# Another order of the loads, the weight splits and the mask copies at the start of a fused linear-attention and feed-forward kernel

## Chip, cores and metric

The kernel runs on one core of a Trainium2 chip. The metric is the device time in microseconds of one execution; lower is better. Times given are medians of several runs.

## The reference

Inputs are q, k, v and f_logit of shape (4, 8, 768, 48), and two pairs of weights, w_in (384, 2048) and w_out (2048, 384), all float32.

```python
# gated linear attention, a recurrence over time t
f = 1 / (1 + exp(-f_logit))
for t in range(S):
    state = f[:, :, t, :, None] * state + einsum('bhd,bhe->bhde', k[:, :, t], v[:, :, t])
    y[:, :, t] = einsum('bhd,bhde->bhe', q[:, :, t], state)
x = y.transpose(0, 2, 1, 3).reshape(B * S, H * D)          # 3072 tokens x 384
# feed-forward layer 1: ELU
h = x @ w_in1;  g = where(h > 0, h, exp(min(h, 0)) - 1);  x = g @ w_out1
# feed-forward layer 2: squared ReLU
h = maximum(x @ w_in2, 0);  out = (h * h) @ w_out2
```

## The kernel before

The sequence is cut into NC = 6 chunks of C = 128 steps. A unit (c, h) is chunk c of two of the four batches (h is 0 or 1), so there are twelve units, each with eight heads per batch. Within a unit the decayed score matrix is built in seven levels l = 0 to 6: product(c, h, l) on TensorE (PE) multiplies keys by queries of neighbouring blocks of width 2**l. After each level the queries and keys are multiplied by running products of the gates (q_update and own_k_update on VectorE, DVE; k_update on GpSimd, POOL; double makes the next products of the gates), and take (DVE, a masked copy, levels 0 to 4) and take5 and take6 (ScalarE, ACT) move the scores from PSUM to the tile PT; in the units of chunk 0 take4 on ACT does level 4. Then come transpose_keys, krow_copy (ACT), new_state (keys times values), q_state (queries times the old state), values (scores times values, padded into vz by pad_v), state_update (DVE) and last_column. Units (0, 0) and (0, 1) come first by themselves, with no feed-forward work beside them, as there is no attention output yet.

The first feed-forward layer works on tiles of 512 tokens in steps f = 0 to 15. hidden(c, f) is nine 512-column matmuls (each float32 operand is held as a high and a low float32r half: three products for three blocks of channels), output(c, f) nine more. Between them: hidden_copies (ACT: Exp into e, Relu into g), activate (DVE), high (ACT, makes ghi) and low (DVE or POOL, makes glo). The attention of chunk c is interleaved with the feed-forward of chunk c - 1 in half-step slots by feed(c, h, slots): first_period and second_period are the two halves for c = 1, period(c, h) the pattern for c = 2 to 5. After that feed_forward runs what is left of layer 1 and layer 2.

Weights of layer 1 come as 32 chunks of 128 x 384, alternately from w_in and w_out. load_weights on SyncE (SP) loads them, split_weights on ACT makes the high half, split_weights on DVE the low half. Chunks 0 to 11 (STAGED) go to the tile stage, which lies where xhi, xlo, e, g and others are later; so first_x_split, which writes xhi, waits for the low halves of all twelve. Later chunks pass through the four buffers of raw, and load_weights waits there for the low half of chunk i - 4. split_at(1, f) says which chunks ACT splits after step f of chunk 1.

Each engine runs its own queue in the order in which its block of the program is written; there is no planner. Semaphores tie them: s_mm counts finished level products, and `level(s_mm, c, h, l)` is the wait for product(c, h, l); s_kT the transposed keys, s_u new_state, s_inter q_state, s_last the last columns. `taken(c, h, n)` is the wait for the first n takes of a unit. For the units from (1, 1) on product(c, h, l) with l = 1 or 2 waits for l takes:

```python
elif l in (1, 2):
    pe.wait_ge(*taken(c, h, l))
```

group(c, h, i) (L1318) on PE is product(c, h, 4 + i) followed by product(c, h + 1, i), where group(1, 1, i) takes the first product of unit (1, 2) as h + 1 = 2.

SP issues all loads of q, k, gates and values. load_v(c, h) loads values for new_state, load_staged_v(c, h) the same values for pad_v. The loads wait for their buffers: load_gates(c, h) for level 0 of unit h - 2 to be done with them, load_k for s_kT, load_q for s_inter, load_v and load_staged_v for s_u.

Of the kernel before, what the change touches and what calls it, by code (L numbers as in the profile page):

```python
# [40 lines left out]
STAGED = 12  # L41
# [60 lines left out]
def attention(nc, blk, sb, sem, ffn, stage, PT, ps, qk, fl, vn, w1, x2, ident_d, mask_d):  # L102
# [47 lines left out]
    s_kT, s_krow = sem("k_transposed"), sem("krow_ready")  # L150
# [9 lines left out]
    def level(sems, c, h, l):  # L160
        if second(c, h):
            return (sems[2], l + 1) if l < EARLY else (sems[3], l - EARLY + 1)
        before = max(2 * c + h - 1, 0)
        if l < EARLY:
            return sems[0], before * EARLY + l + 1
        short = 1 if before and (sems is s_q or sems is s_d) else 0
        return sems[1], before * LATE - short + l - EARLY + 1
# [114 lines left out]
    def more(c, h, n=1):  # L282

        return 2 * c + h + n < UNITS

    @blk.sync
    def _(sp):
        def load_gates(c, h):

            if past(c, h, 2):  # L290
                sp.wait_ge(*level(s_q, c, h - 2, 0))
                sp.wait_ge(*level(s_k, c, h - 2, 0))
                sp.wait_ge(*level(s_d, c, h - 2, 0))
            sp.dma_start(gate[:, h % 2, :].rearrange("p (u n) -> p u n", u=UB),
                         fl[bass.ds(c * B + 2 * h, UB), :, :].rearrange("u p n -> p u n")).then_inc(s_f[h % 2], 16)

        def load_q(c, h):

            if past(c, h, 4):
                sp.wait_ge(s_inter, count(c, h, 1, -3))  # L300
            elif past(c, h, 3):
                sp.wait_ge(*level(s_mm, c, h - 2, LEVELS - 1))
            if past(c, h, 3):
                sp.wait_ge(s_ql, count(c, h, 1, -1))
            for u in range(UB):
                sp.dma_start(queries(c, h)[:, u * PAIRS:(u + 1) * PAIRS, 1:C + 1],
                             qk[bass.ds(c * B + (2 * h + u), 1), :, 0:W]
                             .rearrange("g p (a t) -> p (g a) t", a=PAIRS)).then_inc(s_q_in[h % 2], 16)

        def load_k(c, h):  # L310

            if past(c, h, 3):
                sp.wait_ge(s_kT, count(c, h, 1, -1))
            sp.dma_start(keys_of(c, h).rearrange("p (u n) -> p u n", u=UB),
                         qk[bass.ds(c * B + 2 * h, UB), :, W:2 * W].rearrange("u p n -> p u n")).then_inc(s_k_in[h % 2], 16)

        def load_v(c, h):

            if past(c, h, 2):
                sp.wait_ge(s_u, count(c, h, 1, 0))  # L320
            sp.dma_start(v(c, h), vn[bass.ds(c * B + 2 * h, UB), :, :]
                         .rearrange("u s n -> s u n")).then_inc(s_v[h % 2], 16)

        def load_staged_v(c, h):

            if past(c, h, 2):
                sp.wait_ge(s_u, count(c, h, 1, 0) if past(c, h, 3) else 1)
            for u in range(UB):
                sp.dma_start(staged_v(c, h)[HP * (1 - u):HP * (2 - u), :, :],
                             vn[c * B + (2 * h + u), :, :].rearrange("(z s) n -> s z n", z=2)).then_inc(s_vs[h % 2], 16)  # L330

        def load_weights(chunks):
            for i in chunks:
                if i >= STAGED + 4:
                    sp.wait_ge(s_wlo[i % 2], (i - 4) // 2 + 1)
                sp.dma_start(w1_raw(i), w1[chunk_at(i), :, :]).then_inc(w1_loaded(i)[0], 16)

        def period(c, h):
            if more(c, h, 2):
                load_gates(c, h + 2)  # L340
                load_k(c, h + 2)
                load_q(c, h + 2)
            if more(c, h):
                sp.wait_ge(*level(s_mm, c, h + 1, 4))
                load_v(c, h + 1)
                load_staged_v(c, h + 1)

        def first_period():
            sp.wait_ge(*level(s_mm, 1, 0, 1))
            load_weights(range(18, 20))  # L350
            load_gates(1, 2)
            sp.wait_ge(*level(s_mm, 1, 0, 2))
            load_staged_v(1, 0)
            load_weights(range(20, 22))
            sp.wait_ge(*level(s_mm, 1, 0, 4))
            load_weights(range(22, 24))
            load_v(1, 0)
            sp.wait_ge(*level(s_mm, 1, 1, 1))
            load_gates(1, 3)
            load_weights(range(24, 26))  # L360

        def second_period():
            load_k(1, 2)
            load_q(1, 2)
            load_v(1, 1)
            load_staged_v(1, 1)
            load_weights(range(26, 30))
            sp.wait_ge(*level(s_mm, 1, 2, 0))
            load_weights(range(30, 32))
            load_k(1, 3)  # L370
            load_q(1, 3)
            sp.wait_ge(*level(s_mm, 1, 2, 4))
            load_v(1, 2)
            load_staged_v(1, 2)

        load_q(0, 0)
        sp.dma_start(gate[:, 0, W:2 * W], fl[1, :, :]).then_inc(s_f[0], 16)
        load_q(0, 1)
        sp.dma_start(ident[:], ident_d).then_inc(s_ident, 16)
        sp.wait_ge(*level(s_mm, 0, 0, 0))  # L380
        load_gates(1, 0)
        sp.wait_ge(*level(s_mm, 0, 0, 1))
        load_gates(1, 1)
        load_weights(range(1))
        sp.wait_ge(*level(s_mm, 0, 0, 2))
        load_q(1, 0)
        sp.wait_ge(*level(s_mm, 0, 1, 1))
        load_weights(range(1, 2))
        load_staged_v(0, 0)
        sp.wait_ge(*level(s_mm, 0, 0, 4))  # L390
        load_staged_v(0, 1)
        load_v(0, 0)
        sp.wait_ge(*level(s_mm, 0, 0, 5))
        load_weights(range(2, 4))
        sp.wait_ge(*level(s_mm, 0, 0, 6))
        load_v(0, 1)
        load_k(1, 0)
        load_weights(range(4, 6))
        sp.wait_ge(s_y, 1)
        load_weights(range(6, STAGED))  # L400
        sp.wait_ge(s_last, 1)
        load_weights(range(STAGED, FIRST_SPLIT))
        sp.wait_ge(s_last, 2)
        load_q(1, 1)
        load_k(1, 1)
        load_weights(range(16, 18))
        first_period()
        second_period()
        for c in range(2, NC):
            for h in range(2):  # L410
                period(c, h)

    @blk.scalar
    def _(act):
# [210 lines left out]
                    .to_broadcast([HP, n, X, 32]), ACT.Copy).then_inc(s_mask, 1)  # L625
        gates(0, 1, True)
        gates(1, 0, True)
        gates(1, 1, True)
        split_weights(range(0, 1))
        nc.scalar.activation(warm[:, 1:2], warm[:, 0:1], ACT.Exp)  # L630
        split_weights(range(1, 2))
        pad_v(0, 0)
        take4(0, 0)
        take5(0, 0)
        pad_v(0, 1)
        take4(0, 1)
        take6(0, 0)
        take5(0, 1)
        split_weights(range(2, 4))
        take6(0, 1)  # L640
        krow_copy(0, 0)
        split_weights(range(4, 7))
# [114 lines left out]
    def _(dve):  # L757
# [179 lines left out]
        def first_period():  # L937
# [26 lines left out]
            rest(1, 1, 0)  # L964
            activate(1, 5)
            low(1, 5)
            q_update(1, 0, 5)
            own_updates(1, 1, 1)
            take(1, 1, 1)
            activate(1, 6)  # L970
            double(1, 0, 5)
            double(1, 1, 1)
            low(1, 6)
            q_update(1, 0, 6)
            own_updates(1, 1, 2)
            split_weights(split_at(1, 5))
            activate(1, 7)
            rest(1, 0, 6)
            rest(1, 1, 2)
# [4 lines left out]
        def second_period():  # L984
            activate(1, 8)
            low(1, 8)
            state_update(1, 0)
            activate(1, 9)
            low(1, 9)
            split_weights(split_at(1, 9))  # L990
            activate(1, 10)
            q_update(1, 1, 4)
            own_updates(1, 2, 0)
            low(1, 10)
            rest(1, 1, 4)
            take(1, 2, 0)
            activate(1, 11)
            double(1, 2, 0)
            q_update(1, 1, 5)
            own_updates(1, 2, 1)  # L1000
            low(1, 11)
            take(1, 2, 1)
            activate(1, 12)
            double(1, 1, 5)
            double(1, 2, 1)
            low(1, 12)
            own_updates(1, 2, 2)
            own_k_update(1, 1, 6)
            take(1, 2, 2)
            split_weights(range(28, 29))  # L1010
            activate(1, 13)
            low(1, 13)
            double(1, 2, 2)
            q_update(1, 1, 6)
            double(1, 1, 6)
            step(1, 2, 3)
            activate(1, 14)
            low(1, 14)
            split_weights(range(30, 31))
            state_update(1, 1)  # L1020
            split_weights(range(29, 32, 2))

        nc.vector.memset(e[:, 0, :], 0.0).then_inc(s_warm, 1)
        for which in "YA":
# [740 lines left out]
```

## Time and profile before

| | |
|---|---|
| Time, median of 3 runs | 972.11 us (971.56 to 974.31) |
| Profiled execution, its own time | 971.56 us |
| Its span, first to last instruction | 969.8 us |
| Mean granted clock of TensorE | 0.982 |
| PE busy | 951.4 us (98%), 11636 matmuls |
| DVE busy | 504.0 us (52%) |
| ACT busy | 402.8 us (42%) |
| POOL busy | 236.8 us (24%) |
| Chain that ended last | PE 97%, DMA 1%, DVE 1%, issue 1% |

The table is read as follows. Busy time is the time in which an engine executed; register, branch and DMA-issuing instructions don't count. The chain that ended last is followed back from the last instruction, at each step to what released it. "Issue" is time in which an engine waited for nothing that the profile shows. The granted clock is TensorE's clock as a share of full speed.

### The profile page before, as it was taken

To read this page: it belongs to the slowest core of one execution; us is meant where nothing else is said; L and a number is where in the kernel's file an instruction comes from. 1 tells how busy PE (TensorE), PEld (TensorE's weight loads), DVE (VectorE), ACT (ScalarE), POOL (GpSimd) and SP (SyncE) were. 2 spreads that over 40 slices of the span, in tenths; PEclk is the share of its full clock that TensorE was granted. 3 is DMA by queue.
4 is the path that set the end of the run, shared out by engine and by line. 5 is a ranking of instruction groups with operands and counts; after the bars stand their busy time and mean duration, and the time that the engine had idled before them with its cause. 6 is when DMAs were issued, how large, how long until landed. Compare 5 with 4: busy or idle time off the path is not lost.

```text
span 969.8 us, 27529 instructions
## 1 busy us (share of the span) xinstructions
PE 951.4 (98%) x11636; PEld 785.4 (81%) x11636; DVE 504.0 (52%) x746; ACT 402.8 (42%) x706; POOL 236.8 (24%) x193
## 2 busy tenths in 40 slices
PE   6899999999999999999999999999999999999998
PEld 5778787887887888888878888888888888888897
DVE  7788577576666656572326653343343433433432
ACT  4656545353534543453444452242332422423322
POOL 3102216354545445454424550000000000000000
PEclk6789999999999999999999999999999999999999
DMA  7552312212121211110203331002020030020100
GB/s 238 164 158 91 110 50 86 79 45 79 56 79 45 71 63 57 46 67 3 66 2 122 98 102 37 1 14 53 0 54 11 0 64 1 9 56 0 21 14 33
DMA packets 72428, 56.88 MB, mean 59 GB/s; under 512 B 37249, under 2 KB 64641, under 8 KB 72321
## 3 DMA queue, kind: packets, MB, share of 16 engines
q1 hardware_dynamic: 69472, 43.87, 16.6%
q10 hardware_dynamic: 2848, 11.44, 3.3%
q8 instruction: 85, 1.39, 0.6%
q14 instruction: 23, 0.18, 0.1%
HBM read 45.84 MB, written 9.44 MB: 57 GB/s over the span
## 4 chain that ended last, share of the span: by engine, by line
PE 97%; DMA 1%; DVE 1%; issue 1%; ACT 0%; SPq 0%; DVEq 0%
PE ps L1667 8%; PE ps L1663 8%; PE ps L1662 8%; PE ps L1137 8%; PE ps L1686 7%; PE ps L1682 7%; PE ps L1683 7%; PE ps L1276 6%; PE ps L1299 6%; PE ps L1278 6%; PE ps L1285 6%; PE ps L1301 6%; PE ps L1305 5%; PE ps L1206 2%; PE ps L1172 1%; PE ps L1154 1%
## 5 line engine op out<-in xcount | busy, mean ns | idle before, releaser
L1607 DVE TENSOR_TENSOR g<-g 128x512 f32<-128x512 f32 x96 | 66.8, 696 | 240.9 <-ACT g L1522 240.3
L1522 ACT ACTIVATE g<-ps 128x512 f32<-128x512 f32 x112 | 67.0, 598 | 276.9 <-PE ps L1667 272.6
L688 POOL TENSOR_TENSOR glo<-g,ghi 128x512 fp32r<-128x512 f32 x65 | 89.6, 1379 | 194.3 <-ACT ghi L513 194.3
L1662 PE MATMUL ps<-xhi,wts 128*128 128x512 f32 x336 | 130.9, 390 | 0.0
L1663 PE MATMUL ps<-xhi,wts 128*128 128x512 f32 x336 | 130.9, 390 | 0.0
L872 DVE SCALAR_TENSOR_TENSOR g<-e,g 128x512 f32<-128x512 f32 x80 | 57.8, 723 | 136.7 <-ACT g L507 136.7
L1682 PE MATMUL ps<-ghi,wts 128*128 128x512 f32 x294 | 114.4, 389 | 0.0
L1683 PE MATMUL ps<-ghi,wts 128*128 128x512 f32 x294 | 114.4, 389 | 0.0
L506 ACT ACTIVATE e<-ps 128x512 f32<-128x512 f32 x80 | 47.8, 598 | 158.7 <-PE ps L1285 158.7
L1276 PE MATMUL ps<-xhi,wts 128*128 128x512 f32 x240 | 98.9, 412 | 0.2 <-ACT g L507 0.2
L1278 PE MATMUL ps<-xhi,wts 128*128 128x512 f32 x240 | 94.7, 395 | 0.3 <-issue 0.3
L1667 PE MATMUL ps<-xlo,wts 128*128 128x512 f32 x336 | 94.6, 390 | 0.0
L1299 PE MATMUL ps<-ghi,wts 128*128 128x512 f32 x234 | 93.8, 401 | 0.0
L1618 DVE TENSOR_TENSOR glo<-g,ghi 128x512 fp32r<-128x512 f32 x112 | 89.3, 798 | 5.6 <-ACT ghi L1529 5.1
L1301 PE MATMUL ps<-ghi,wts 128*128 128x512 f32 x234 | 91.3, 390 | 0.0
L1686 PE MATMUL ps<-glo,wts 128*128 128x512 f32 x294 | 82.8, 390 | 0.0
L1137 PEld LDWEIGHTS ps<-q,k 48*63 48x63 f32 (+6 forms) x4576 | 68.6, 134 | 17.4 <-issue 16.3
L1137 PE MATMUL ps<-q,k 48*63 48x32 f32 (+6 forms) x4576 | 74.7, 219 | 1.3 <-DVE PT L828 1.1
L1667 PEld LDWEIGHTS ps<-xlo,wts 128*128 128x128 f32 x336 | 63.1, 188 | 13.5 <-DVE xlo L865 0.3
L1662 PEld LDWEIGHTS ps<-xhi,wts 128*128 128x128 f32 x336 | 63.0, 188 | 13.1 <-ACT xhi L498 0.2
L513 ACT ACTIVATE ghi<-g 128x512 fp32r<-128x512 f32 x80 | 50.5, 631 | 55.6 <-DVE g L872 55.5
L1663 PEld LDWEIGHTS ps<-xhi,wts 128*128 128x128 f32 x336 | 63.1, 188 | 12.6
(132 smaller groups left out, 1555.8 us busy)
## 6 DMA issues: line engine op xcount, KB each, us to landing
raw<-w SPq DMA_DIRECT2D x52, 192.0 KB, 2.4
q<-qk SPq DMA_DIRECT2D x22, 256.0 KB, 3.7
gate<-fl SPq DMA_DIRECT2D x10, 512.0 KB, 4.4
k<-qk SPq DMA_DIRECT2D x10, 512.0 KB, 3.7
x<-xo ACTq DMA_DIRECT2D x6, 768.0 KB, 3.3
xs<-x ACTq DMA_DIRECT2D x6, 768.0 KB, 4.4
v<-vn SPq DMA_DIRECT2D x11, 384.0 KB, 3.6
krow<-vn SPq DMA_DIRECT2D x20, 192.0 KB, 4.5
```

The costliest lines, as they stand in the source:

```text
L688: nc.gpsimd.tensor_tensor(out=glo[:, f % 2, :], in0=g[:, f % 2, :], in1=ghi[:, f % 2, :].bitcast(F32), op=ALU.subtract).then_inc(s_glo, 1)
L1137: last = nc.tensor.matmul(to, k_all[rows, at * C + HP * z:at * C + HP * z + m], there, start=True, stop=True)
L1276: nc.tensor.matmul(ps[:, HID, :], wts[:, f, 0, m * P:(m + 1) * P], xhi[:, m, :], start=(m == 0), stop=False)
L1278: nc.tensor.matmul(ps[:, HID, :], wts[:, f, 1, m * P:(m + 1) * P], xhi[:, m, :], start=False, stop=False)
L1299: nc.tensor.matmul(ps[:, ACC + m, :], wts[:, n, 0, m * P:(m + 1) * P], ghi[:, f % 2, :], start=start, stop=False)
L1301: nc.tensor.matmul(ps[:, ACC + m, :], wts[:, n, 1, m * P:(m + 1) * P], ghi[:, f % 2, :], start=False, stop=False)
L1662: nc.tensor.matmul(h, w(0, k), xhi[:, k, :], start=(k == 0), stop=False)
L1663: nc.tensor.matmul(h, w(1, k), xhi[:, k, :], start=False, stop=False)
L1667: last = nc.tensor.matmul(h, w(0, k), xlo[:, k, :], start=False, stop=(k == KD - 1))
L1682: nc.tensor.matmul(acc[m], w(0, m), ghi[:, f % 2, :], start=start, stop=False)
L1683: nc.tensor.matmul(acc[m], w(1, m), ghi[:, f % 2, :], start=False, stop=False)
L1686: last = nc.tensor.matmul(acc[m], w(0, m), glo[:, f % 2, :], start=False, stop=stop)
```

## The change

Four functions get another order. No instruction is added or removed, apart from waits.

- SP, the opening: the twelve staged chunks are loaded in pairs from product(0, 0, 1) on; before, chunks 0 and 1 were loaded early, 2 to 5 about the ends of unit (0, 0)'s levels, and 6 to 11 after unit (0, 0)'s values. q and k of unit (1, 0) come after the last levels.
- SP, first_period: staged values and values of unit (1, 0) first, gates of unit (1, 2) after product(1, 0, 3) instead of product(1, 0, 1).
- SP, second_period and period: the wait for level 4 of the next unit ahead of load_v is gone, and load_q comes behind the values.
- ACT, the opening: chunks 0 to 3 are split earlier.
- DVE, first_period: chunks 22 and 23 are split after low(1, 5), not after own_updates(1, 1, 2); take(1, 1, 1) comes after activate(1, 6), not before.
- DVE, second_period: chunks 28 and 29 are split before activate(1, 11); take(1, 2, 1) comes after activate(1, 12), not before; 30 and 31 are split before low(1, 13), not at the end. (rest is take, where the level has one on DVE, and then double.) For unit (1, 2) level 0, take and double now both come before activate(1, 11).

```diff
--- before.py
+++ after.py
@@ -336,25 +336,27 @@
                 sp.dma_start(w1_raw(i), w1[chunk_at(i), :, :]).then_inc(w1_loaded(i)[0], 16)
 
         def period(c, h):
+            f = 8 * h
             if more(c, h, 2):
                 load_gates(c, h + 2)
+            if more(c, h, 2):
                 load_k(c, h + 2)
-                load_q(c, h + 2)
             if more(c, h):
-                sp.wait_ge(*level(s_mm, c, h + 1, 4))
                 load_v(c, h + 1)
                 load_staged_v(c, h + 1)
+            if more(c, h, 2):
+                load_q(c, h + 2)
 
         def first_period():
             sp.wait_ge(*level(s_mm, 1, 0, 1))
+            load_staged_v(1, 0)
             load_weights(range(18, 20))
+            sp.wait_ge(*level(s_mm, 1, 0, 2))
+            load_v(1, 0)
+            load_weights(range(20, 22))
+            sp.wait_ge(*level(s_mm, 1, 0, 3))
             load_gates(1, 2)
-            sp.wait_ge(*level(s_mm, 1, 0, 2))
-            load_staged_v(1, 0)
-            load_weights(range(20, 22))
-            sp.wait_ge(*level(s_mm, 1, 0, 4))
             load_weights(range(22, 24))
-            load_v(1, 0)
             sp.wait_ge(*level(s_mm, 1, 1, 1))
             load_gates(1, 3)
             load_weights(range(24, 26))
@@ -368,10 +370,9 @@
             sp.wait_ge(*level(s_mm, 1, 2, 0))
             load_weights(range(30, 32))
             load_k(1, 3)
-            load_q(1, 3)
-            sp.wait_ge(*level(s_mm, 1, 2, 4))
             load_v(1, 2)
             load_staged_v(1, 2)
+            load_q(1, 3)
 
         load_q(0, 0)
         sp.dma_start(gate[:, 0, W:2 * W], fl[1, :, :]).then_inc(s_f[0], 16)
@@ -380,24 +381,29 @@
         sp.wait_ge(*level(s_mm, 0, 0, 0))
         load_gates(1, 0)
         sp.wait_ge(*level(s_mm, 0, 0, 1))
+        load_weights(range(0, 2))
+        sp.wait_ge(*level(s_mm, 0, 0, 2))
+        load_staged_v(0, 0)
         load_gates(1, 1)
-        load_weights(range(1))
-        sp.wait_ge(*level(s_mm, 0, 0, 2))
-        load_q(1, 0)
-        sp.wait_ge(*level(s_mm, 0, 1, 1))
-        load_weights(range(1, 2))
-        load_staged_v(0, 0)
+        sp.wait_ge(*level(s_mm, 0, 0, 3))
+        load_weights(range(2, 4))
+        sp.wait_ge(*level(s_mm, 0, 1, 2))
+        load_weights(range(4, 6))
         sp.wait_ge(*level(s_mm, 0, 0, 4))
         load_staged_v(0, 1)
+        load_weights(range(6, 7))
+        sp.wait_ge(*level(s_mm, 0, 1, 3))
+        load_weights(range(7, 9))
+        sp.wait_ge(*level(s_mm, 0, 0, 5))
+        load_weights(range(9, 10))
         load_v(0, 0)
-        sp.wait_ge(*level(s_mm, 0, 0, 5))
-        load_weights(range(2, 4))
-        sp.wait_ge(*level(s_mm, 0, 0, 6))
+        sp.wait_ge(*level(s_mm, 0, 1, 4))
+        load_weights(range(10, STAGED))
+        sp.wait_ge(*level(s_mm, 0, 1, 5))
         load_v(0, 1)
+        load_q(1, 0)
+        sp.wait_ge(s_kT, 1)
         load_k(1, 0)
-        load_weights(range(4, 6))
-        sp.wait_ge(s_y, 1)
-        load_weights(range(6, STAGED))
         sp.wait_ge(s_last, 1)
         load_weights(range(STAGED, FIRST_SPLIT))
         sp.wait_ge(s_last, 2)
@@ -625,18 +631,18 @@
                     .to_broadcast([HP, n, X, 32]), ACT.Copy).then_inc(s_mask, 1)
         gates(0, 1, True)
         gates(1, 0, True)
+        split_weights(range(0, 2))
         gates(1, 1, True)
-        split_weights(range(0, 1))
         nc.scalar.activation(warm[:, 1:2], warm[:, 0:1], ACT.Exp)
-        split_weights(range(1, 2))
         pad_v(0, 0)
+        split_weights(range(2, 3))
         take4(0, 0)
+        split_weights(range(3, 4))
         take5(0, 0)
         pad_v(0, 1)
         take4(0, 1)
         take6(0, 0)
         take5(0, 1)
-        split_weights(range(2, 4))
         take6(0, 1)
         krow_copy(0, 0)
         split_weights(range(4, 7))
@@ -964,16 +970,15 @@
             rest(1, 1, 0)
             activate(1, 5)
             low(1, 5)
+            split_weights(split_at(1, 5))
             q_update(1, 0, 5)
             own_updates(1, 1, 1)
-            take(1, 1, 1)
             activate(1, 6)
-            double(1, 0, 5)
-            double(1, 1, 1)
+            rest(1, 0, 5)
+            rest(1, 1, 1)
             low(1, 6)
             q_update(1, 0, 6)
             own_updates(1, 1, 2)
-            split_weights(split_at(1, 5))
             activate(1, 7)
             rest(1, 0, 6)
             rest(1, 1, 2)
@@ -993,32 +998,29 @@
             own_updates(1, 2, 0)
             low(1, 10)
             rest(1, 1, 4)
-            take(1, 2, 0)
+            rest(1, 2, 0)
+            split_weights(split_at(1, 10))
             activate(1, 11)
-            double(1, 2, 0)
+            low(1, 11)
             q_update(1, 1, 5)
             own_updates(1, 2, 1)
-            low(1, 11)
-            take(1, 2, 1)
             activate(1, 12)
-            double(1, 1, 5)
-            double(1, 2, 1)
+            rest(1, 1, 5)
+            rest(1, 2, 1)
             low(1, 12)
             own_updates(1, 2, 2)
             own_k_update(1, 1, 6)
             take(1, 2, 2)
-            split_weights(range(28, 29))
             activate(1, 13)
+            split_weights(split_at(1, 12))
             low(1, 13)
             double(1, 2, 2)
             q_update(1, 1, 6)
-            double(1, 1, 6)
+            rest(1, 1, 6)
             step(1, 2, 3)
             activate(1, 14)
             low(1, 14)
-            split_weights(range(30, 31))
             state_update(1, 1)
-            split_weights(range(29, 32, 2))
 
         nc.vector.memset(e[:, 0, :], 0.0).then_inc(s_warm, 1)
         for which in "YA":
```

## Rows read from the trace of the kernel before

**Rows 1.** Waits of PE, 55 us on: sum, count, longest (longest of four).

```profile
PE ps L1206 <- issue: 0.5, 1, 0.5
```

**Rows 2.** Timeline of PE: start, us, line, operation, count, idle before.

```profile
31.98 0.69 PE L1137 MATMUL ps<-xo,xs 48*64 48x64 f32 x12 [1.22 <-issue]
...
42.63 0.93 PE L1245 MATMUL ps<-g,e 128*48 128x48 f32 x32 [0.75 <-ACT e L469]
...
45.61 2.54 PE L1259 MATMUL ps<-q_last,state 128*64 128x1 f32 x64
```

**Rows 3.** Timelines of ACT (first two, last) and DVE, 41 to 48 us.

```profile
41.14 0.53 ACT L484 ACTIVATE wts<-stage 128x384 fp32r<-128x384 f32 x1 [0.92 <-DMA stage<-w]
...
41.57 1.00 ACT L469 ACTIVATE e<-ps 128x1024 f32<-128x1024 f32 x1
...
46.10 1.03 DVE L851 TENSOR_TENSOR wts<-stage,wts 128x384 fp32r<-128x384 f32 x2 [0.31 <-ACT wts L484]
...
47.22 1.88 ACT L490 ACTIVATE xhi<-ps 128x384 fp32r<-128x384 f32 x4 [0.67 <-DVE wts L851]
```

**Rows 4.** Timeline of ACT: take5(0, 0).

```profile
28.40 1.20 ACT L455 ACTIVATE PT<-ps 32x512 f32<-32x512 f32 x2 [0.24 <-PE ps L1137]
```

**Rows 5.** Timeline of PE: products, and where feed-forward blocks begin.

```profile
48.09 1.93 PE L1137 MATMUL ps<-q,k 48*63 48x32 f32 x64
...
49.94 0.79 PE L1276 MATMUL ps<-xhi,wts 128*128 128x512 f32 x1
...
53.83 1.11 PE L1137 MATMUL ps<-q,k 48*62 48x32 f32 x64
...
55.16 0.47 PE L1276 MATMUL ps<-xhi,wts 128*128 128x512 f32 x1 [0.23 <-ACT g L507]
...
57.32 0.39 PE L1299 MATMUL ps<-ghi,wts 128*128 128x512 f32 x1
```

**Rows 6.** Stretches: PE busy, its granted clock, DMA (first: all engines).

```profile
40.00:45.00 5.00, 3.24 (x141) 2.39 (x136) 4.51 (x9) 2.92 (x6) 0.00 (x0) 1.00 0.75 223
...
46.50:47.00 0.50, 0.50 (x18) 0.65 0.11 33
...
53.00:53.50 0.50, 0.50 (x2) 0.52 1.09 358
```

**Rows 7.** Timelines of DVE and PE, 84 to 87 us.

```profile
84.64 1.30 DVE L828 COPY_PREDICATED PT<-mask,ps 128x512 f32<-128x512 uint8 x1
...
86.23 1.55 PE L1137 MATMUL ps<-q,k 48*64 48x64 f32 x96
```

**Rows 8.** Timelines of DVE, ACT and PE, 117 to 124 us.

```profile
117.87 0.70 DVE L872 SCALAR_TENSOR_TENSOR g<-e,g 128x512 f32<-128x512 f32 x1
...
119.09 1.54 DVE L781 TENSOR_TENSOR q<-q,decay_late 128x512 f32<-128x512 f32 x1
...
121.76 0.68 DVE L880 TENSOR_TENSOR glo<-g,ghi 128x512 fp32r<-128x512 f32 x1
...
122.37 1.30 DVE L828 COPY_PREDICATED PT<-mask,ps 128x512 f32<-128x512 uint8 x1
...
119.15 1.18 ACT L455 ACTIVATE PT<-ps 32x512 f32<-32x512 f32 x2
...
120.35 0.94 ACT L443 ACTIVATE vz<-krow 128x384 f32<-128x384 f32 x2
...
122.22 0.59 ACT L507 ACTIVATE g<-ps 128x512 f32<-128x512 f32 x1
...
123.66 1.55 PE L1137 MATMUL ps<-q,k 48*64 48x64 f32 x96
```

**Rows 9.** Timelines of PE, ACT; then the page's DMA issues.

```profile
66.81 1.03 PE L1137 MATMUL ps<-q,k 48*56 48x32 f32 x64
...
74.58 1.06 ACT L419 ACTIVATE gate<-gate 128x1024 f32<-128x1024 f32 x1
...
gate<-fl SPq DMA_DIRECT2D x10, 512.0 KB, 4.4
```

## The prediction

> **What bounds the kernel now.** I read the waits of TensorE (PE) first, then its timeline over the opening, then the timelines of the engines that feed it. After 55 us PE waits only four times in more than 900 us, 1.2 us in all, and the longest wait is 0.5 us [rows 1]. The span is PE work laid end to end, so no transfer and no VectorE (DVE) or ScalarE (ACT) step is worth anything there unless PE is made to wait for it. Before 50 us PE does wait: the reader should see a gap of 1.22 us with no releaser (the profile calls it issue), and one of 0.75 us before new_state(0, 1), released by ACT's copy of the transposed keys into e [rows 2]. The change can thus win only in the opening; after it, it can win nothing and lose wherever a reordered step comes late.
>
> **The opening: staged weights earlier.** In the old order ACT stands at a staged weight that has not landed (idle 0.92 us), splits it at 41.14, and only then makes krow_copy(0, 1), 41.57 to 42.57, for which PE waits until 42.63 [rows 2, 3]. The new SyncE (SP) order issues chunks 4 to 11 during the level products, all before load_v(0, 1), instead of after unit 0's levels. ACT then finds them there, krow_copy(0, 1) runs about a microsecond earlier or more, and PE's 0.75 us are gone: -0.75. What is late next? DVE makes four low halves, then state_update(0, 1), then four more low halves, the last pair at 46.10 for 1.03 us, of which only 0.31 us was a wait for ACT; ACT's first_x_split follows at 47.22 [rows 3]. That DVE chain holds its place and moves up by only about 0.3 us; it ends near 46.8, ACT's four pieces 1.9 us later, at 48.7. PE's own order (last columns 45.61 to 48.15, product(1, 0, 0) 48.09 to 50.0, first hidden block 49.94 [rows 2, 5]) arrives at 49.2 when moved up by 0.75, so DVE and ACT stay just ahead of it. I take -0.7. The ends: -1.4, if PE is fed ever so little better and the other short gaps go too, and +1.2, one more gap of the size of that at 31.98.
>
> The moved ACT work there: chunks 0 and 1 are split before gates(1, 1), 2 and 3 around take4(0, 0). Each split is about 0.5 us, and ACT has idle time at DMA waits ahead of them; the step that PE needs is take5(0, 0), which waited for PE itself, 0.24 us [rows 4]. Nominally hidden, up to +0.5 if gates(1, 1), now queued behind load_staged_v(0, 0), lands late. load_q(1, 0) and load_k(1, 0) are issued near 34 and 36 for a product at 47: nothing.
>
> **TensorE's clock.** It falls to the lower of its two levels (1.2 GHz instead of 2.4) inside the half microsecond from 46.5, and is back after 53.0 [rows 6]. The price is readable: product(1, 0, 0) takes 1.93 us and product(1, 0, 1), at full clock, 1.11; the first hidden block runs from 49.94 to 53.83, 3.9 us, the second from 55.16 to 57.32, 2.2 us [rows 5]. So the low stretch costs 0.8 + 1.7 = 2.5 us. Before the fall came 40 to 45 us, of which PE was busy 3.24, and then 2.54 us of matmuls with one column each [rows 2, 6]. The change removes one of these waits and none of the one-column matmuls, so I take 0 and keep -2.5 as an end.
> The Trainium skill (TensorE: Matmul & The Clock Gate, "What's actually happening") has the clock fall only after the engine was idle. The trace does not agree: in the half microsecond where it fell PE was busy throughout [rows 6]. By that rule, read with the trace's small idle times, removing 0.75 us could well keep the clock up, and the sum below would be 2.5 us lower.
>
> **First period (steps 0 to 7 of the feed-forward).** DVE now splits chunks 22 and 23 right after low(1, 5), two times 0.51 us by the pair in [rows 3], ahead of q_update(1, 0, 5); and take(1, 1, 1), which ran from 84.64, ahead of activate(1, 6), now comes behind it and behind double(1, 0, 5) [rows 7]. A step follows the next after about 0.6 us (0.61 from low to take in [rows 8]). So take(1, 1, 1) starts at 84.64 + 1.02 + 0.60 + 0.1 = 86.36 and, at 1.1 us before the next step could start, ends at 87.46. PE starts this group at 86.23 with the 32 matmuls of product(1, 0, 6), a third of a group of 1.55 us, and asks for take(1, 1, 1) at 86.75, before product(1, 1, 2). Wait: 0.7 us. Queued behind it on PE are hidden(1, 7) and all the rest, and no slack exists to give it back, so +0.7. Ends: 0 and 1.6, the latter if a DVE step there is drawn out by 0.9 us, as the q_update of 1.54 us was [rows 8]. The later place of the old split (before activate(1, 7)) is freed, which only brings the order back to where it was.
>
> **Second period.** Here DVE gets chunks 28 and 29 ahead of activate(1, 11), and take(1, 2, 1), formerly done at 123.46, is moved behind activate(1, 12). In [rows 8] activate(1, 11) started at 117.87. Now double(1, 2, 0) (0.6) and the two splits (1.0) come first, so it starts at 119.5 and ends, with the drawn-out 0.9 us that one step has at that spot in the old order too, at about 121.0. Everything on ACT waits for it: high(1, 11) to 121.5, take5(1, 1) 1.2, pad_v 0.9, then hidden_copies(1, 12), whose Relu (formerly 122.22 to 122.8) now ends at 124.7. activate(1, 12) ends at 125.3, double(1, 1, 5) at 125.4, take(1, 2, 1) at 126.5. PE starts group(1, 1, 2) at 123.66 and reaches product(1, 2, 2), which waits for that take, at 124.2 [rows 8]. Wait: 2.3 us, with hidden(1, 13) queued behind it. Ends: 0.4 us, if activate(1, 11) is fast enough for ACT to keep its old times (Relu at 122.8, then 0.6 + 0.1 + 1.1 gives 124.6), and 3.2 us with one more drawn-out step. Steps further on (take(1, 2, 2), the split of 30 and 31, take(1, 2, 3)) fall behind by less than this wait gives back.
>
> **SP's other moves.** gates(1, 2) now wait for product(1, 0, 3), issued at 66.81 and done at 67.8, instead of product(1, 0, 1). A load of gates was 4.4 us on its way (median), so it lands near 72.3; ACT reads it at 74.58, just before high(1, 4) [rows 9]. Cost 0; were it 2.3 us later still, ACT would hold back ghi(1, 4), on which the whole of PE would wait. load_v and load_staged_v ahead of load_q, without the wait for the next unit's level 4, send the values some 8 us sooner, and load_q still waits only for q_state of its own unit, a microsecond after new_state. No wait in [rows 1] names a DMA: 0 for all ten periods.
>
> **Sum.** Profiled execution 971.56 us (span 969.8 plus 1.8 around it): -0.7 + 0.7 + 2.3 = +2.3, so 973.9. The profiled run is the fastest of three and 0.55 us below their median of 972.11, so I forecast a median of 974.4.
>
> **Rivals.**
> 1. The clock falls once more. Condition: the wait at 124 us, of some 2 us, is enough for it; the point from which it decides is a PE idle time there like the 1.76 us that is missing between 40 and 45 us [rows 6], after which it fell. Price: the low stretch lasted 6.5 us [rows 6], half of which is lost in dense work, 3.3 us. Time 977.7. For: the fall of [rows 6] needed no long idle. Against: the matmuls around 124 us are 512 columns wide. It would be slower.
> 2. The waits come, at their long ends, or PE's issue gaps in the opening grow because the weights now share the DMA rings with them: 1.6 + 3.2 - 0.7 = +4.1, or +2.3 + 1.2 + 0.5 = +4.0: 976.1. For: the 1.22 us gap stands right behind heavy transfers. Against: these gaps are few.
> 3. The clock stays up in the opening: -0.7 - 2.5 + 3.0 = -0.2, 971.9, within the noise.
> 4. The reordered steps are absorbed (DVE had idle time here and there that the shift eats) and the clock stays up: -1.4 - 2.5 + 0.4 = -3.5, 968.6. It needs both; for it speaks only that the old order has several DVE waits for ACT, against it that these takes must follow a Relu which itself follows PE.
> The Trainium skill (GPSIMD Engine Reference, "1. Specifications") says that GpSimd shares its SBUF interfaces with VectorE. The stretched 1.54 us step agrees in kind; without the sharing the second wait would be about 1.4 us and the sum 0.9 us lower.
>
> **Chances.** Forecast 0.42; rival 1 0.18; rival 2 0.17; rival 3 0.12; rival 4 0.11. What a measurement tells from no change is 0.3%, 2.9 us. Forecast and rival 3 lie within it except for the forecast's upper tail (0.05): faster 0.12, same 0.48, slower 0.40. Range: 968.9 (nearly rival 4) to 978.5 (rival 1 with 0.8 us more); the likeliest case alone runs from 972.5 to 976.
>
> **What would show it.** Right: no ACT idle time for stage weights before krow_copy(0, 1), first hidden block near 49.2, a PE wait of about 0.7 us near 86 released by the masked copy into PT, one of about 2 us near 123 likewise. Wrong: no PE wait after 55 us, a first hidden block later than 50, a granted clock below full after 60 us, or a PE wait for ACT's ghi near 78 (the gates).

## The result, and the profile after

The changed kernel takes 979.97 us (median of 5, 978.26 to 981.43) against 972.11: ratio 1.0074, interval 1.0054 to 1.0092. It is slower by 7.2 us by this ratio; the medians lie 7.9 apart. I had forecast 974.4, no difference that can be measured. In a second comparison, below, the ratio was 1.0083 (1.0067 to 1.0099). The profiled execution took 977.67 us.

Of the page: the span, PE's busy time, and the chain that ended last.

```profile
span 975.9 us, 27520 instructions
...
PE 953.0 (98%) x11636; PEld 786.8 (81%) x11636; DVE 504.7 (52%) x746; ACT 402.1 (41%) x706; POOL 237.8 (24%) x193
...
PE 94%; DVE 2%; issue 2%; ACT 1%; DMA 1%; SPq 0%; DVEq 0%; ACTq 0%
```

PE is busy 1.6 us longer than before, but the span grew by 6.1: PE now waits. Before, nothing above 0.5 us held it up after 55 us [rows 1]. Now the timeline of PE (start, length, line, operation, count; in brackets the idle time before and what ended it) shows these, beside the gap in the opening:

```profile
43.34 0.98 PE L1228 MATMUL ps<-PT,vz 64*64 64x64 f32 x48 [2.58 <-issue]
...
50.91 0.80 PE L1278 MATMUL ps<-xhi,wts 128*128 128x512 f32 x1
...
75.67 0.43 PE L1139 MATMUL ps<-q,k 48*63 48x32 f32 x17 [1.17 <-issue]
...
89.83 1.08 PE L1139 MATMUL ps<-q,k 48*60 48x32 f32 x64 [0.70 <-DVE PT L834]
...
130.03 1.08 PE L1139 MATMUL ps<-q,k 48*60 48x32 f32 x64 [2.39 <-DVE PT L834]
...
150.41 1.48 PE L1139 MATMUL ps<-q,k 48*48 48x32 f32 x95 [1.35 <-issue]
```

Read the bracket. The waits of 0.70 and 2.39 us are released by DVE's masked copy into PT: the two that I forecast, with 0.7 and 2.3 us. The three others have no releaser ("issue"), and two of them stand in the middle of a product (17 of a group's 128 matmuls follow one, 95 of 128 the other), where the program has no wait at all. The first hidden block begins at 50.91 us (49.94 before, [rows 5]; I had forecast 49.2), though PE no longer waits for the copy that held it up in [rows 2]. The four of them after 60 us come to 5.6 us, 5.9 with one of 0.29 at 320, against 1.0 us in the kernel before; with the opening's 1.0 us that is 5.9 of the span's 6.1.

TensorE's clock was at its half level in the opening again, in two pieces, for as long as in the kernel before. PE's busy time, granted clock, DMA share and GB/s of these stretches, the kernel before first:

```profile
46.60:53.40 6.80, 6.80 (x112) 0.50 0.77 211
```

```profile
44.00:47.40 3.40, 3.40 (x108) 0.51 0.02 5
...
50.80:54.20 3.40, 3.40 (x10) 0.51 0.93 248
```

The mean granted clock of the whole span, 0.996 against 0.982, says nothing of the change. It differs by a stretch from about 9 to 36 us, in which the clock was at half level in six of the twelve profiles without padding, both of the kernel before among them, and full in the other six. It seems to cost nothing there: from 10 to 30 us the kernel before at half level and the changed one at full level both had 644 matmuls on PE.

How the second wait comes about, on DVE and ACT of the changed kernel, to be laid beside [rows 8]:

```profile
119.75 1.30 DVE L834 COPY_PREDICATED PT<-mask,ps 128x512 f32<-128x512 uint8 x1
...
121.50 1.86 DVE L857 TENSOR_TENSOR wts<-raw,wts 128x384 fp32r<-128x384 f32 x2
...
123.28 0.68 DVE L878 SCALAR_TENSOR_TENSOR g<-e,g 128x512 f32<-128x512 f32 x1
...
124.53 1.19 ACT L461 ACTIVATE PT<-ps 32x512 f32<-32x512 f32 x2
...
125.75 0.94 ACT L449 ACTIVATE vz<-krow 128x384 f32<-128x384 f32 x2
...
127.21 0.59 ACT L513 ACTIVATE g<-ps 128x512 f32<-128x512 f32 x1
...
127.90 0.69 DVE L878 SCALAR_TENSOR_TENSOR g<-e,g 128x512 f32<-128x512 f32 x1 [0.74 <-ACT g L513]
...
128.60 1.29 DVE L834 COPY_PREDICATED PT<-mask,ps 128x512 f32<-128x512 uint8 x1
```

The two splits (1.86 us here, one of them drawn out), activate(1, 11), then ACT's take5 and pad_v, the Relu of step 12, activate(1, 12), and last the masked copy of take(1, 2, 1) for which PE stands: the order of my reckoning. take(1, 2, 0), the first row, is 3.0 us later than in the kernel before; the start of take(1, 2, 1) at 128.60 was reckoned at 125.4, and 3.0 on that is 128.4.

The first wait came about in part otherwise than reckoned. DVE there, to be laid beside [rows 7]:

```profile
83.65 1.88 DVE L857 TENSOR_TENSOR wts<-raw,wts 128x384 fp32r<-128x384 f32 x2
...
87.68 0.69 DVE L878 SCALAR_TENSOR_TENSOR g<-e,g 128x512 f32<-128x512 f32 x1 [0.34 <-ACT g L513]
...
88.38 1.30 DVE L834 COPY_PREDICATED PT<-mask,ps 128x512 f32<-128x512 uint8 x1
```

The two splits took 1.88 us, not 1.02, and DVE still waited 0.34 us for ACT's Relu before activate(1, 6). So by this trace the wait comes from the take's place behind activate(1, 6), and not from the splits ahead of it.

### The profile page after: what moved, and what is told of

Read it like the earlier page. It is cut to its first block, busy times and chain, and to the rows that moved or that the text cites. A ratio compares the mean times of both kernels' runs of the same rounds, so it can differ in the third digit from the quotient of the medians.

```text
span 975.9 us, 27520 instructions
## 1 busy us (share of the span) xinstructions
PE 953.0 (98%) x11636; PEld 786.8 (81%) x11636; DVE 504.7 (52%) x746; ACT 402.1 (41%) x706; POOL 237.8 (24%) x193
## 4 chain that ended last, share of the span: by engine, by line
PE 94%; DVE 2%; issue 2%; ACT 1%; DMA 1%; SPq 0%; DVEq 0%; ACTq 0%
PE ps L1669 8%; PE ps L1665 8%; PE ps L1664 8%; PE ps L1139 7%; PE ps L1688 7%; PE ps L1684 7%; PE ps L1685 7%; PE ps L1278 6%; PE ps L1301 6%; PE ps L1280 5%; PE ps L1287 5%; PE ps L1303 5%; PE ps L1307 5%; PE ps L1208 2%; PE ps L1156 1%
## 5 line engine op out<-in xcount | busy, mean ns | idle before, releaser
L519 ACT ACTIVATE ghi<-g 128x512 fp32r<-128x512 f32 x80 | 50.5, 631 | 55.8 <-DVE g L878 55.7
```

## The experiments

The first four split the change. Times of the kernel before differ a little from call to call, so ratios are against the runs of the same call. A difference in microseconds is that of the medians, unless it is said to be by the ratio.

**VectorE's order alone** (dve_only), first_period and second_period of DVE as in the change:

```diff
             low(1, 5)
+            split_weights(split_at(1, 5))
             q_update(1, 0, 5)
             own_updates(1, 1, 1)
-            take(1, 1, 1)
             activate(1, 6)
-            double(1, 0, 5)
-            double(1, 1, 1)
+            rest(1, 0, 5)
+            rest(1, 1, 1)
...
```

> The kernel before with only VectorE's new order in first_period and second_period. Theory (the masked copies late by their place in VectorE's order): the profile has PE waits released by the masked copy into PT of about 0.7 us near 87 us and 2.4 us near 124 us, the opening and all else as before; time 3.1 us above the kernel before. Rival (the waits come about only together with the new loads, whose traffic or later weights draw VectorE out): waits under half of that, time within 1.5 us of the kernel before.

Measured: 977.67 us, ratio 1.0052 (1.0033 to 1.0070), 6.0 us above before (5.1 by the ratio), where 3.1 was expected. The waits themselves are as expected, 0.78 and 2.39 us. What else there is shows in stretches (PE busy, its granted clock, DMA share, GB/s):

```profile
126.00:129.00 3.00, 0.90 (x34) 1.00 0.02 5
...
130.00:133.00 3.00, 3.00 (x36) 0.50 0.00 0
...
134.00:140.00 6.00, 6.00 (x91) 1.00 0.09 18
```

Behind the wait PE is busy all the time, at half its clock, the 1.2 GHz level. This low stretch lasts about 3.4 us and costs 1.7, half of it, as PE is busy throughout. Most of the rest of the profile's difference is an issue gap of 0.71 us near 251 and an opening 1.2 us later; that gap is in profiles with DVE's old order too, and the opening's end differs by more than that between them (below).

**Loads and ScalarE's splits alone** (loads_only), DVE as before:

```diff
-                sp.wait_ge(*level(s_mm, c, h + 1, 4))
                 load_v(c, h + 1)
                 load_staged_v(c, h + 1)
+            if more(c, h, 2):
+                load_q(c, h + 2)
...
```

> The kernel before with only the new orders of SyncE's loads and of ScalarE's weight splits in the opening; VectorE as before. Theory (PE's instruction fetch queues behind bursts of loads): no PE wait for the masked copy, but issue gaps of PE of about 2.6 us near 41 to 43 us (0.76 before), 1.2 us near 75 and 1.3 us near 146; first hidden block near 50.9; time 3 to 4 us above the kernel before. Rival (the gaps come from the later VectorE order or differ from run to run by chance): gaps in the profile like those of before, the first hidden block near 49.2, time at or below the kernel before.

Measured: 974.3 us, ratio 1.0027 (1.0014 to 1.0040), 2.6 us above before. No PE wait for the masked copy after 60 us; issue gaps of 2.06 us near 41, 0.71 at 74 and 1.00 at 145. The first block began at 50.20. So the theory has it, with smaller gaps than in the first profile and a cost a little under the 3 to 4 us expected.

**The opening alone** (open_only): SP's order up to s_last, and ACT's early splits.

```diff
...
+        sp.wait_ge(*level(s_mm, 0, 1, 2))
+        load_weights(range(4, 6))
...
         load_v(0, 1)
+        load_q(1, 0)
+        sp.wait_ge(s_kT, 1)
         load_k(1, 0)
```

> The kernel before with only the opening's loads and ScalarE splits changed. Theory of the fetch behind a burst: the issue gap near 41 to 43 us is there with about 2.6 us, the ones near 75 and 146 are not; first hidden block near 50.9; time about 1 us above before. Rival (my forecast's reckoning of the opening): gap near 41 as before with 0.8 us, first hidden block near 49.2, time 0.7 us below before.

Measured: 972.51 us, ratio 1.0009 (0.9995 to 1.0023): no difference. The gap near 41 us is 1.96 us, the wait for the key copy is gone. My -0.7 did not come, nor quite the +1 of the theory: one gap grew by about what the other wait gave.

**The loads of the later periods alone** (period_only):

```diff
-                sp.wait_ge(*level(s_mm, c, h + 1, 4))
                 load_v(c, h + 1)
...
-            load_q(1, 3)
-            sp.wait_ge(*level(s_mm, 1, 2, 4))
             load_v(1, 2)
             load_staged_v(1, 2)
+            load_q(1, 3)
```

> The kernel before with only the loads of second_period and period changed (no wait for the next unit's level 4 ahead of load_v, and load_q behind the values). Theory of the fetch behind a burst: an issue gap of PE of about 1.3 us in the product near 144 us, nothing in the opening, time about 1.3 us above before. Rival (the gap belongs to something else in the new kernel, such as a page of instructions that ends elsewhere): no such gap, time as before.

Measured: 974.51 us, ratio 1.0020 (1.0005 to 1.0035), 2.8 us above before, 1.9 by the ratio. The gap is there, 1.07 us, in the middle of product(2, 0, 4), and the clock fell behind it for 3.4 us. Another, 1.43 us, stands at 246. PE's timeline:

```profile
143.46 1.48 PE L1138 MATMUL ps<-q,k 48*48 48x32 f32 x95 [1.07 <-issue]
...
246.46 0.65 PE L1138 MATMUL ps<-q,k 48*62 48x32 f32 x29 [1.43 <-issue]
```

**The order of first_period's loads alone** (first_only):

```diff
             sp.wait_ge(*level(s_mm, 1, 0, 1))
+            load_staged_v(1, 0)
             load_weights(range(18, 20))
+            sp.wait_ge(*level(s_mm, 1, 0, 2))
+            load_v(1, 0)
+            load_weights(range(20, 22))
+            sp.wait_ge(*level(s_mm, 1, 0, 3))
             load_gates(1, 2)
...
-            sp.wait_ge(*level(s_mm, 1, 0, 4))
             load_weights(range(22, 24))
-            load_v(1, 0)
```

> The kernel before with only SyncE's order in first_period changed (gates of unit (1, 2) and chunks 22 and 23 loaded after product(1, 0, 3)). Theory of the fetch behind a burst: an issue gap of PE of 0.7 to 1.2 us in the product near 74 us, all else as before; time 0.7 to 1 us above before. Rival (the gap at 75 us needs the other parts): no gap, time as before.

Measured: 971.96 us, ratio 1.0003 (0.9992 to 1.0014), and no gap near 74. A miss for the theory in this form. The gap near 75 is in all four profiles that have this order together with the new opening (1.17, 0.89, 0.71, 0.89 us) and in none of the others: it needs both. The packets of PE's instructions, read below, show how near it was: here the one for this place started at 70.0 us, just ahead of the burst of loads, in the four others behind it. Why the opening matters 25 us later is open.

**PE's instructions moved by 48** (period_pad12 and before_pad12). Twelve idle matmuls in the opening, on top of the loads of period_only and on the kernel before:

```diff
         keep_warm(2)
+        for _ in range(12):
+            nc.tensor.matmul(ps[:, PAIR_Y, 0:1], e[:, 0, 0:P], e[:, 0, 0:1], start=True, stop=True)
```

> The kernel with only the loads of second_period and period changed, plus 12 one-column matmuls on PE in the opening, where PE waits for the first queries. They do nothing but move every later block of PE's instructions by 48 instructions. Theory (the gap of 1.07 us near 143 us is a fetch of a block of instructions that falls into a burst of loads): the block ends some 5 us earlier against the loads, so the gap near 143 is gone or much smaller, and so is the one of 1.43 at 246 or it changes; time 1 to 3 us below that kernel's 974.5. Rival (the gap comes from the loads' effect on the data that PE waits for): gap at the same product, same size; time as before the padding.

> The kernel before plus the same 12 one-column matmuls. Theory of the fetch: its issue gaps of the opening (1.22 us at 31, 0.76 at 41, 0.67 at 45) move to other instructions and change size, most of them to places with other traffic; time within 1.5 us of before, no sign forecast. Rival (those gaps are semaphore waits that the profile does not show): same gaps at the same instructions.

Measured: 978.32 us (1.0074, 1.0056 to 1.0093) and 980.9 (1.0094, 1.0075 to 1.0112). Both are far above what was expected, but the times are no test: the padding took 5.1 us in the profile of before_pad12 and 3.1 in the other, where PE had only 1.7 to spare, and in both the first hidden block began near 55.8, six microseconds late. The places of the gaps are a test. Here are the gaps of the padded kernel before (first two rows) and of the padded period_only:

```profile
34.67 0.37 PE L1137 MATMUL ps<-q,k 48*48 48x32 f32 x3 [0.82 <-issue]
...
159.60 0.81 PE L1137 MATMUL ps<-q,k 48*62 48x32 f32 x21 [1.37 <-issue]
```

```profile
32.85 0.37 PE L1138 MATMUL ps<-q,k 48*48 48x32 f32 x3 [1.93 <-issue]
...
159.29 0.53 PE L1138 MATMUL ps<-q,k 48*62 48x32 f32 x21 [1.01 <-issue]
```

A float32 matmul is two rows in the trace, so 24 went in. In the kernel before, the gap at 31.98 stood after 20 matmuls of product(0, 0, 6) [rows 2]. Now there is one after 61 of the 64 matmuls of the product before it: 23 rows earlier. The gaps at 143 and 246 of period_only are gone, though the same loads stand in the same order there; others stand at 159 and 456. The one at 159 has 3376 rows of PE ahead of it in both padded profiles, and so has one of 0.30 to 0.63 us in four of those without padding: the same place in the count, 24 rows earlier in the program. A wait for a semaphore would stay with its instruction. These gaps go by the count of instructions, which points to waits for PE's own instructions, and these come by DMA in blocks: the queue table of 66 to 72 us has one 16 KB packet of the instruction queue in the kernel before, and none in the changed one, whose gap comes at 74.5:

```profile
q1 hardware_dynamic: 269, 0.36, 19.3%
...
q8 instruction: 1, 0.02, 1.0%
```

```profile
q1 hardware_dynamic: 569, 0.92, 48.3%
```

What is in its place is 0.92 MB of loads instead of 0.36. The same holds from 36 to 40.8 us: one block fetched before, none after.

The packets show it directly. In the kernel before the block for this place started at 70.7 us; in the changed one it started at 73.3, when the burst was over, and the gap ended at 75.67. Here are the stretch ahead of it in the kernel before, then of the changed kernel the burst, the stretch behind it, and the queue in that last stretch:

```profile
68.00:70.60 2.60, 2.60 (x12) 1.00 0.00 0
```

```profile
70.50:73.20 2.70, 2.70 (x37) 1.00 0.89 328
...
73.20:74.30 1.10, 1.10 (x103) 1.00 0.07 22
```

```profile
q8 instruction: 1, 0.02, 5.4%
```

All twelve profiles without padding have 51 issue gaps of PE of 0.6 us or more. They stand at ten places in its count of rows, and each of them ends 1.16 to 1.61 us after such a packet has landed (in the padded ones 10 of 12; the two at row 668 don't, and are not explained). The packets ahead of the gaps near 75 and 143 to 152 us took 0.9 to 1.1 us, hardly more than elsewhere: they started late. In the 2 us before their start the DMA engines' busy share was 0.82 to 1.13; at the same places in the profiles without a gap it was at most 0.61. The gaps near 245 are another matter. Their packets also started late (with 4925 to 4993 rows of PE done, against 4901 to 4922 without a gap), but with a share of 0.43 or less ahead of them, so no burst explains these.
The Trainium skill (Runtime: NRT & Kernel Launch, "Instruction fetch mechanics") calls the crossing of a 16 KiB boundary mostly hidden; most crossings here agree (85 packets of that queue in the changed kernel, seven issue gaps above 0.15 us), gaps of up to 2.58 us behind loads do not.

**One load of the opening moved back** (open_q_early):

```diff
         load_gates(1, 1)
+        load_q(1, 0)
...
         load_v(0, 1)
-        load_q(1, 0)
```

> The kernel with only the opening's new order, with one load moved back: the queries of unit (1, 0), 512 KB, are loaded right after the gates of unit (1, 1), near 17 us, instead of between the values and the keys near 34 us. Theory (the issue gap of 2 us at 40 us is a fetch of PE instructions behind the burst of values, queries and keys that starts at 34 us): gap at 40 us down to 0.8 to 1.2 us, first hidden block near 49.2, time 0.5 to 1 us below the kernel before. Rival (another load or the weights make the gap): 2 us as in the opening alone, time as before.

Measured: 971.73 us, ratio 1.0000 (0.9990 to 1.0010). Waits of PE up to 60 us in both, open_only first; the line with L1231 is values(0, 0) and (0, 1), where the gap near 41 is:

```profile
PE ps L1142 <- issue: 2.0, 3, 1.2
...
PE ps L1231 <- issue: 2.0, 1, 2.0
```

```profile
PE ps L1142 <- issue: 3.8, 3, 1.8
...
PE ps L1231 <- issue: 1.1, 2, 0.8
```

The gap is 0.76 us again, in the range of the old opening: this load, where the change puts it, does make the gap near 41 long. But the level products' gaps went from 2.0 to 3.8 us in this profile; that the load now lies among their fetches is my reading, and not shown. The first block was at 49.96, not near 49.2, and the expected gain of 0.5 to 1 us did not come.

**The key copy first, no load moved** (krow_first):

```diff
         krow_copy(0, 0)
-        split_weights(range(4, 7))
         krow_copy(0, 1)
-        split_weights(range(7, STAGED))
+        split_weights(range(4, STAGED))
```

> The kernel before with krow_copy(0, 1) ahead of the splits of chunks 4 to 11 on ScalarE, and no load moved. Theory of my forecast (removing PE's wait of 0.75 us before new_state(0, 1) moves the opening up by as much): that wait is gone, first hidden block near 49.2, time 0.7 us below before, unless the later splits, which still wait for the loads, set the end; then they do, and the first block stays at 49.9 (the rival).

Measured: 972.33 us, ratio 1.0003 (0.9990 to 1.0016). The wait is gone and the first block is at 50.42: an issue gap at 46 stands at 1.49 us (0.67 before). The forecast's reasoning about the opening, that PE's end moves up by the wait that is removed, fails here without any load moved.

**One take moved back** (take_back), in the changed kernel:

```diff
             own_updates(1, 2, 1)
+            take(1, 2, 1)
             activate(1, 12)
             rest(1, 1, 5)
-            rest(1, 2, 1)
+            double(1, 2, 1)
```

> The changed kernel with one step moved back: take(1, 2, 1) ahead of activate(1, 12), as in the kernel before; the early split of chunks 28 and 29 stays. Theory (the wait at 127 us comes from the take's place behind a Relu that follows PE, and the early splits add some): the PE wait there goes from 2.39 us to about 0.8 us, too short for the clock to fall behind it; the waits near 87 (0.7), 75 and 149 us stay; time 1.6 us below the changed kernel, more (up to 3.3) if the clock falls behind that wait in some of its executions. Rival (the early splits alone make the wait): still about 2 us of waiting, time as the changed kernel's, 980.

Measured: 976.55 us, ratio 1.0045 (1.0029 to 1.0062), 3.4 us below the changed kernel. PE's wait there is 0.87 us:

```profile
127.22 1.08 PE L1140 MATMUL ps<-q,k 48*60 48x32 f32 x64 [0.87 <-DVE PT L834]
```

The saving is more than twice the 1.5 us of waiting removed, which fits a clock that often fell behind the long wait; with intervals of some 1.6 us on either time it does not prove it. The 0.87 us that are left with the take back in its place come from the other moves, the splits ahead of activate(1, 11) among them. In this profile the clock fell behind two issue gaps, not behind this wait.

**Both kernels once more** (after_again, before_again), unaltered.

> The changed kernel once more, unaltered, for a second profile. Theory (its median lies 2 us above its first profiled execution because the clock falls for a while behind one of its new waits in most executions, and an issue gap near 250 us comes in some): PE waits of 0.7 and 2.4 us for the masked copy again, gaps near 75 and 149 of 0.7 to 1.4 us, and a stretch at half clock behind one of them; span 977 to 979. Rival (the first profile is typical and the clock stays up): span 976, clock full after 60 us.

> The kernel before once more, unaltered, for a second profile: how much the opening and the gaps differ from run to run with nothing changed. Theory: second hidden block between 54.5 and 56.5 us, no PE wait for the masked copy, issue gaps after 60 us under 0.5 us except perhaps one near 245; time 971.5 to 972. Rival: issue gaps near 75 and 144 here too, which would make them no work of the change.

Measured: 979.84 us (1.0083, 1.0067 to 1.0099) and 972.2 (1.0003, 0.9992 to 1.0014). The changed kernel has waits of 0.70 and 2.36 us again, gaps of 0.89 and 0.67 at 75 and 152, and this behind the second wait, in the same columns as above:

```profile
125.00:128.00 3.00, 1.81 (x38) 1.00 0.02 5
...
129.00:135.00 6.00, 5.82 (x74) 0.50 0.00 0
...
136.00:140.00 4.00, 4.00 (x83) 1.00 0.01 4
```

Six microseconds and more at half clock with PE 5.82 us busy, where the first profile had full clock. The kernel before, unaltered, shows an issue gap too, and a low stretch behind it:

```profile
243.10 0.65 PE L1137 MATMUL ps<-q,k 48*62 48x32 f32 x29 [1.16 <-issue]
...
244.50:247.00 2.50, 2.50 (x8) 0.50 0.00 0
```

So the gap near 245 is no work of the change; it is in six of the twelve profiles without padding, the first of before not among them. Nor is a first hidden block as late as 50.91 us: it began between 48.69 and 51.18 us in the five profiles with the old opening, and between 49.71 and 50.91 in the five with the new one.

The gap near 41, of the size 0.18 to 1.03 us in the five profiles with the old opening and 0.55 with only the key copy moved, is 1.58 to 2.58 in the five with the new one. The gap of 0.67 to 1.35 near 143 to 152 is in all five with the new period loads and in none of the seven without them, four of which have one of 0.30 to 0.63 us at 154 to 160.

## Why the prediction was wrong, point by point

- What bounds the kernel (PE, end to end after 55 us): right.
- First period, 0.7 us, and second period, 2.3 us: right, 0.70 to 0.78 and 2.36 to 2.39 in the three profiles that have VectorE's new order whole. In the second the steps between came as reckoned. In the first the size is right in part by luck: the splits that I had added to the chain took 0.86 us more than I put in and yet did not set it.
- TensorE's clock in the opening, 0: right in sum, 6.8 us at half level in either kernel.
- TensorE's clock behind the new wait: this step failed. I priced the clock only where it had been seen and gave a new fall behind the second wait as rival 1, chance 0.18 and 3.3 us. It came in two of three profiles with that wait, at 1.7 us (3.4 us low) and 3.4 us (6.8 us low), so it belonged in the sum, at some 1.7 us on average. The clocks of all executions agree with that, not only the profiled ones. Leaving out those with the early stretch at half level (mean 0.984 or less), the changed kernel's mean granted clock averages 0.9939 over 8 executions, and before's 0.9959 over the 27 of the second comparison; 0.002 of the span is 2.0 us. By dve_only against its waits, 5.1 or 6.0 against 3.2 us, a third to a half of what VectorE's order costs is not the waits themselves.
- SP's other moves, "0 for all ten periods": this step failed too, and cost as much. I had looked at whether a load would be late for its reader, and not at what it delays: PE's own instructions. The gaps at 75 and 150 us came to 2.5 us in the first profile and 1.6 in the second; all the loads together cost 2.6 us by their own run. The gates themselves came in time; no PE wait for ghi is in the profile. I had this mechanism in rival 2 but only for the opening, with 1.2 us.
- The signs that I had named for being wrong: the first profile has one, a first hidden block later than 50 us; after_again adds a clock below full after 60 us.
- The opening, -0.7 us: wrong. The wait for the key copy went, as said, and a fetch gap grew by as much. open_only and krow_first both came out at no difference.

By the ratios, VectorE's order with 5.1 and the loads with 2.6 make 7.7 us, against 7.2 and 8.1 measured for the whole; the intervals of the parts, 1.3 to 1.8 us each way, cover the rest. Against the forecast, VectorE's order was 2.1 us dearer than its +3.0, and the loads with the opening 3.3 dearer than their -0.7. Why the clock falls behind one wait of 2.4 us and stays up behind another is not settled, nor what the opening has to do with the gap at 75.

## What to carry to other kernels

On an engine that bounds the kernel, price a new wait by its length and by what the clock does behind it: here a wait of 2.4 us took the clock along in two of three profiles. Before moving a load to a "free" time, look where the bounding engine fetches its next block of instructions, visible as gaps with no releaser in the middle of a loop without waits, each a little more than a microsecond behind a packet of the instruction queue. A step that ends just before its reader asks has no slack, however idle its engine is on average.

## What the runs showed of the hardware

PE's gaps without a releaser move with the number of instructions ahead of them (24 rows of matmuls in, gap 23 rows earlier), end 1.16 to 1.61 us after a 16 KB packet of the instruction queue has landed, and three of the places have longer ones where loads of some 1 MB are issued just ahead: near 41 us (1.58 to 2.58 against 0.18 to 1.03), near 75 (0.71 to 1.17 against none) and near 143 to 152 (0.67 to 1.35 against none). TensorE's clock fell to its half level for 3.4 us behind gaps of 0.9 to 1.5 us in the profiles before_again (1.16), first_only (0.92), krow_first (1.47), period_only (1.07 and 1.43) and take_back (1.07 and 1.47), and stayed up in others behind 1.35 and 2.39 us.
